# Two last products of a block in the other order, in a scan and MoE kernel on one core

## What is computed

```python
sig = 1 / (1 + exp(-f_logit));  f = lb + (1 - lb) * sig;  i = 1 - f
h = 0
for t in range(S):                 # S = 6080, batch 2, width 256
    h = f[:, t] * h + i[:, t] * x[:, t]
    y[:, t] = h
h = y.reshape(12160, 256) @ w_in   # 256 x 2048
g = h * clip(h + 3, 0, 6) / 6
return g @ w_out                   # 2048 x 256
```

## Time and profile before

| what | value |
|---|---|
| median of 3 runs | 1106.84 us (1103.45 to 1106.91) |
| the profiled execution | 1102.24 us, of which its span is 1100.5 us |
| busy share of PE, DVE, ACT, POOL | 93%, 78%, 67%, 21% |
| mean granted TensorE clock | 0.977 |

### The profile page before, as it was taken

How to read it: one execution, slowest core, us unless ns; L and a number is a source line. 1 busy time by engine, 2 the same in 40 slices (tenths; PEclk the granted TensorE clock), 3 DMA queues, 4 the chain that set the end, 5 groups by cost and what they waited for, 6 DMA issues and landing times.

```text
span 1100.5 us, 12941 instructions
## 1 busy us (share of the span) xinstructions
PE 1018.1 (93%) x4356; PEld 823.4 (75%) x4356; DVE 861.7 (78%) x1190; ACT 739.8 (67%) x1229; POOL 232.0 (21%) x176
## 2 busy tenths in 40 slices
PE   2788999998999999999899899999999999989998
PEld 2566787887777787787777778777778778777886
DVE  7687779788779778768778868877977886887675
ACT  3666676776776677676677677577767667766765
POOL 5655402202201301311210220220130121022000
PEclk7899999999999999999999999999999999999999
DMA  6200030030030030011003003003002000200000
GB/s 224 72 1 1 1 113 1 1 113 1 1 116 1 1 115 1 0 42 74 1 1 115 1 0 115 1 1 115 1 1 94 22 1 13 103 1 1 39 1 39
DMA packets 12707, 42.39 MB, mean 39 GB/s; under 512 B 1376, under 2 KB 1376, under 8 KB 12640
## 3 DMA queue, kind: packets, MB, share of 16 engines
q1 hardware_dynamic: 12640, 41.56, 10.4%
HBM read 29.10 MB, written 12.45 MB: 38 GB/s over the span
## 4 chain that ended last, share of the span: by engine, by line
DVE 35%; PE 30%; ACT 18%; issue 13%; DMA 2%; POOL 1%; SPq 0%; ACTq 0%; DVEq 0%; POOLq 0%
DVE g L479 14%; DVE g_lo L484 9%; ACT g_hi L339 8%; ACT g L332 6%; PE y_ps L587 5%; PE y_ps L588 5%; PE y_ps L589 5%; DVE h_sb L461 5%; PE x_ps L566 3%; PE x_ps L568 3%; PE x_ps L570 3%; DVE x_sb L426 3%; DVE x_sb L440 3%; DMA x_sb<-in_x 2%; PE v_ps L566 2%
## 5 line engine op out<-in xcount | busy, mean ns | idle before, releaser
L339 ACT CAST g_hi<-g 128x512 fp32r<-128x512 f32 (+1 forms) x384 | 233.9, 617 | 147.8 <-DVE g L479 146.3
L479 DVE SCALAR_TENSOR_TENSOR g<-g,h_sb 128x512 f32<-128x512 f32 (+1 forms) x288 | 230.6, 801 | 101.0 <-ACT g L332 99.0
L587 PE MATMUL y_ps<-g_hi,w_out_hi 128*128 128x512 f32 (+1 forms) x768 | 300.2, 391 | 0.3 <-DVE g_lo L484 0.3
L588 PE MATMUL y_ps<-g_lo,w_out_hi 128*128 128x512 f32 (+1 forms) x768 | 300.2, 391 | 0.0
L589 PE MATMUL y_ps<-g_hi,w_out_lo 128*128 128x512 f32 (+1 forms) x768 | 299.7, 390 | 0.0
L332 ACT ACTIVATE g<-h_sb,half 128x512 f32<-128x512 f32 (+1 forms) x288 | 207.4, 720 | 128.0 <-DVE h_sb L461 126.4
L484 DVE TENSOR_TENSOR g_lo<-g,g_hi 128x512 fp32r<-128x512 f32 (+1 forms) x384 | 261.2, 700 | 38.6 <-ACT g_hi L339 15.0
L566 PE MATMUL x_ps<-op_hi,w_hi 128*128 128x512 f32 (+1 forms) x384 | 154.2, 402 | 36.8 <-ACT h_sb L311 25.0
L587 PEld LDWEIGHTS y_ps<-g_hi,w_out_hi 128*128 128x128 f32 x768 | 145.5, 190 | 30.7 <-DVE g_lo L484 0.8
L589 PEld LDWEIGHTS y_ps<-g_hi,w_out_lo 128*128 128x128 f32 x768 | 145.7, 190 | 29.5
L588 PEld LDWEIGHTS y_ps<-g_lo,w_out_hi 128*128 128x128 f32 x768 | 145.5, 189 | 29.6
(11 more groups left out here) (64 smaller groups left out, 1202.1 us busy)
## 6 DMA issues: line engine op xcount, KB each, us to landing
z_sb<-in_z SPq DMA_DIRECT2D x20, 512.0 KB, 6.2
x_sb<-in_x SPq DMA_DIRECT2D x20, 512.0 KB, 7.1
out_y<-y_sb SPq DMA_DIRECT2D x9, 1024.0 KB, 5.3
w_raw<-in_w_in SPq DMA_DIRECT2D x8, 256.0 KB, 7.5
w_out_raw<-in_w_out SPq DMA_DIRECT2D x8, 256.0 KB, 7.5
z_sb<-in_z SPq DMA_DIRECT2D x4, 480.0 KB, 4.4
x_sb<-in_x SPq DMA_DIRECT2D x4, 480.0 KB, 5.6
out_y<-y_sb SPq DMA_DIRECT2D x2, 960.0 KB, 5.3
```

Source lines behind the costliest of these rows:

```text
L339: nc.scalar.copy(g_hi[:, u, 0:n], g[:, u, 0:n]).then_inc(g_hi_ready[u], 1)
L479: nc.vector.scalar_tensor_tensor(g[:, u, 0:n], g[:, u, 0:n], 1.0, h, ALU.min, ALU.mult).then_inc(g_ready[u], 1)
L587: nc.tensor.matmul(out, w_out_hi[:, f, at], g_hi[:, u, 0:n], start=opens, stop=False)
L588: nc.tensor.matmul(out, w_out_hi[:, f, at], g_lo[:, u, 0:n], start=False, stop=False)
```

## The change

```diff
                 if q > 0:
                     down(q - 1, C22, 1).then_inc(down_done[C22], 1)
                     down(q - 1, C21, 0)
+                pe.wait_ge(p165_copied, q + 1)
+                product(q, S4_B22, bank, False, n).then_inc(c12_ready, 1)
+                if q > 0:
+                    down(q - 1, C21, 1).then_inc(down_done[C21], 1)
                 pe.wait_ge(h_ready[C22], q + 1)
                 product(q, A22_T4, v_ps, False, n).then_inc(p74_ready, 1)
-                if q > 0:
-                    down(q - 1, C21, 1).then_inc(down_done[C21], 1)
-                pe.wait_ge(p165_copied, q + 1)
-                product(q, S4_B22, bank, False, n).then_inc(c12_ready, 1)
                 if q > 0:
                     down_both(q - 1, C12)
```

## The result

The changed kernel takes 1132.91 us (median of 4 runs, 1130.27 to 1133.49) against 1105.14 us (4 runs): a ratio of 1.0249, with a 95% interval from 1.0218 to 1.0279. It is slower by some 28 us. The traced execution has a span of 1131.7 us, 31.2 more than the one before. Most of the gap between 28 and 31.2 comes from the trace before: its execution took 1102.24 us, 2.9 less than the median of that kernel.

The account below looks back on a forecast made before the run. PE or DVE sets the pace by block, with a loop through PE, DVE and ACT nearly as long. Terms 11.9 + 6.6 + 2.3 + 1.0 = 21.8 us on 1102.24 give 1124.0, rounded up to 1125 us; range 1115 to 1142.

Parts of the forecast that it names:

- The slack of the loop: S2_T2, A22_T4, `add_c21`, ACT, `copy_p1`, next S2_T2: 0.50 us slack, 1.36 us added, so 11.07 us blocks in place of 10.20.
- S4_B22 earlier helps nobody: S4_B22 two groups earlier on PE: no gain, since clip and gate of C12 stand behind those of C21.
- its wait for `copy_p165` costs nothing: S4_B22's new wait on PE in block 5: free, since A22_T4 waits for `add_c22` until 627.25 anyway.
- The wait for `add_c22` is a symptom: PE's 39.4 us wait before A22_T4: DVE sets the pace in blocks 3 to 5, so removing it gains nothing.
- Rival (b): Not slower: PE's wait for `add_c22` is a true bound, so work ahead of it saves 42 us, giving 1060; chance 0.06.
- The sum over a tile: Eight blocks from S2_T2 to S2_T2 sum to 89.88 us; tiles 2 to 10 together cost +11.9 us.
- In block 7: POOL's operation meets gate C21 on the loop: 11.07 us plus up to 0.57, taken as 0.46.
- Block 0 is open: Block 0 leaves its roundings to block 1, so `copy_p1` is not behind them; PE sets 10.31 us.
- No low clock in tiles 2 to 10: No wait there over 1.2 us, so none of the six low-clock episodes of 1.56 us each remains.
- Rival (a): PE's clock falls more often: one episode in each of tiles 1 to 11 gives 1142 us, two give 1159; chance 0.13.
- Tile 0: Paced by weight splitting on ACT and POOL, covering most of the delay: +1 us, with 0 and 5 as bounds.

Follow-up runs that it names:

- s4_one_earlier: Against the kernel before: S4_B22 one group earlier on PE, A22_T4 in its old place; 1104.81 us, ratio 1.0006.
- copy_first: Against the changed kernel: ACT copies P1 of the next block ahead of the roundings of C21 and C12; 1104.68 us, ratio 1.0009 to the kernel before.
- spread_old: Against the kernel before, PE's order kept: DVE's next-tile work spread over blocks 2 to 6, most ACT casts a block later; 1062.50 us, ratio 0.9615.
- changed_rest_first: Against the changed kernel: in tile 0 DVE takes the rest of C22 ahead of `add_c21`; 1127.10 us against 1132.91.
- only_tile0: Against the kernel before: the changed order on PE in tile 0 alone; 1110.21 us, ratio 1.0043; traced again, 1108.93 us.

## Why the prediction was right, and where it was short

The direction, the mechanism and the range held: 1132.9 us in 1115 to 1142. The size was short, mostly in tile 0. I forecast 21.8 us on the traced execution, and it was 31.2; by medians 28 us against some 20.

- **The slack of the loop, 0.50 us, and its new length.** Right. Predicted 11.07 us for blocks of tile 11, measured 11.10 to 11.11 from S2_T2 to S2_T2. The 3.96 us from `add_c21` to S2_T2 did not move. The waits at S2_T2 show as 0.60 us of idle time in most blocks, not about 0.8.
- **S4_B22 earlier helps nobody, and its wait for `copy_p165` costs nothing.** Right. The wait shows in blocks 5 as predicted, about 0.36 us of idle time where PE would wait for `add_c22` anyway, and s4_one_earlier and tile 11 of copy_first time the earlier product at nothing.
- **The wait for `add_c22` is a symptom.** Right. It fell by 37 us and nothing was gained. Rival (b) falls: work put ahead of the wait is not time gained where the engine waited for is the bound. The sentence that the prediction set beside it (the Trainium skill, "Perfetto Trace Analysis", section "Optimization Strategy") is not refuted by this: it asks for an earlier end of what PE waits for, and this change gives none. spread_old does give it, with PE's order kept: the wait for `add_c22` falls to 7.6 us and 42 us are gained.
- **The sum over a tile.** 89.88 us predicted, 90.14 measured. Block by block in tile 6, from S2_T2 to S2_T2, predicted and measured: 10.31 and 10.37, 10.96 and 10.97, 11.07 and 11.23, 11.07 and 11.09, 11.20 and 11.31, 12.67 and 12.65, 11.07 and 11.12, 11.53 and 11.42. In block 7 it is not gate C21 that meets POOL, as I had it, but the step ahead of it, the rest of C22 (1.30 us in place of 0.69): the size came out near by luck. Block 0 is open as I said, since its roundings stand behind `copy_p1`; copy_first makes all blocks so.
- **No low clock in tiles 2 to 10.** Right: 1.00 over all nine. Rival (a) did not come in them. In these tiles PE's waits of 0.60 us in most blocks, and of 0.94 in blocks 0 and 6, left the clock at its full level. (The waits that the prediction puts at 0.8 us in block 4 before are 0.63 in the trace; the clock was full behind them too.)
- **Tile 0: the term that was mis-sized.** I gave it +1 us, 5 at most, "and the others have more cover". The cover was counted up to ACT's clip of C21 only. What I did not look at is what stands on DVE between `add_c21` and gate C21: the rest of C22, which so far ended 0.23 us before POOL's L216 began. Moved by a microsecond it starts beside it and takes 2.57 us in place of 0.66, and the gate behind it then meets POOL's next operation. The tile measured +6.9, of which changed_rest_first takes 5.4 back. The other 2 to 3 us that were missing are tiles 2 to 10 (+14.2 for +11.9) and tile 1 (+3.1 for +2.3), in amounts of about 0.1 us in some blocks (0.16 in block 2). No run takes these apart.

## What to carry to other kernels

Before work is moved ahead of a wait, ask who reads the product that gets later, and follow it until it comes back to the engine that waited: the slack of that loop, not the length of the wait, says what the move costs. A wait that goes away is no gain where the engine that was waited for is itself the bound; take work from that engine in those blocks instead (here 42 us for a new layout of its list and of ACT's casts). And when a step moves by less than its cover, look along its own engine for the neighbours that move with it, and at what they will then stand beside.

## What the runs showed of the hardware

Steps of DVE whose two inputs are in SBUF wait as a whole for an operation of POOL that has begun before them, and do not share with it: 0.65 us becomes 2.4 to 2.6, ending about 0.5 us behind POOL's end (92.94 + 2.13 = 95.07, and DVE's L484 ends at 93.01 + 2.57 = 95.58). Where DVE is first, its step keeps its 0.65 us and POOL's grows from 2.1 to about 2.5 (2.41 to 2.55 in four blocks of the two only_tile0 traces). The Trainium skill says the same ("SBUF — State Buffer", section "SBUF: two separate sides"): the pair of ports that both engines use is locked for a whole instruction, and whoever starts first has it. The trace agrees in both directions. What I had not expected is that two such steps in a row can each wait out one operation of POOL (2.57 and 1.71 us), and that starts 0.02 us apart can decide it, so that the same block of one kernel takes 14.90 us in one execution and 13.56 in another (block 2 of tile 0 in the two only_tile0 traces, from S2_T2 to S2_T2).
